# Small inverse transform's four short matmuls: in a row, or one by one between the long matmuls of the first MLP's second layer

## What is computed

```python
X = np.fft.rfft(x, axis=1)                       # x: 4 x 3008 x 256
y = np.fft.irfft(X * (filt_r + 1j * filt_i), n=3008, axis=1)
x = y.reshape(12032, 256)
h = np.maximum(x @ moe_w_in, 0.0)                # 256 x 2048
x = (h * h) @ moe_w_out                          # 2048 x 256
g = x @ moe2_w_gate                              # 256 x 1536
out = (g / (1 + np.exp(-g)) * (x @ moe2_w_val)) @ moe2_w_out
```

## Time and profile before

| what | value |
|---|---|
| median of 3 runs | 2360.11 us (2357.04 to 2362.37) |
| the profiled execution's own time | 2358.64 us |
| its span, first to last instruction | 2356.8 us |
| around the span | 1.84 us |
| mean granted TensorE clock | 0.997 of full speed |
| PE busy | 2329.5 us, 99% of the span |
| PEld busy | 1903.6 us, 81% |
| DVE busy | 1601.1 us, 68% |
| ACT busy | 1272.7 us, 54% |
| s4 jobs | 122, between 94.8 us and 1208.3 us of the span |

### The profile page before, as it was taken

One profiled execution on the slowest core, in us unless ns is written; L12 is line 12 of the kernel. 1 busy time (PEld: TensorE's weight loads), 2 busy tenths in 40 slices (PEclk: granted clock), 3 DMA queues, 4 the chain that ended last, 5 costly groups with the idle time before them and its releaser, 6 DMA issues.

```text
span 2356.8 us, 31292 instructions
## 1 busy us (share of the span) xinstructions
PE 2329.5 (99%) x10581; PEld 1903.6 (81%) x10581; DVE 1601.1 (68%) x2707; ACT 1272.7 (54%) x2468; POOL 61.2 (3%) x124
## 2 busy tenths in 40 slices
PE   8899999999999999999999999999999999999999
PEld 4688888888888888888888878888888888888887
DVE  3567766677666776566555777777777777777776
ACT  4566656566655665555544445555555555555554
POOL 0100000000000000000000000000000000000000
PEclk9899999999999999999999999999999999999999
DMA  9643433333333333101002101001011011010000
GB/s 270 207 132 96 129 96 107 91 107 112 101 98 99 99 106 122 29 27 42 27 19 72 50 1 36 23 14 36 1 36 36 1 36 36 1 36 28 10 19 18
DMA packets 95423, 153.74 MB, mean 65 GB/s; under 512 B 10080, under 2 KB 48416, under 8 KB 94976
## 3 DMA queue, kind: packets, MB, share of 16 engines
q1 hardware_dynamic: 82112, 132.96, 17.9%
q0 software_dynamic: 13152, 18.78, 3.3%
HBM read 101.89 MB, written 49.81 MB: 64 GB/s over the span
## 4 chain that ended last, share of the span: by engine, by line
PE 96%; DMA 2%; SPq 1%; ACT 1%; issue 1%; DVE 1%; POOL 0%; ACTq 0%; DVEq 0%
PE psum L1450 31%; PE psum L1452 31%; PE psum L1451 31%; PE psum L1552 1%; DMA filt0b<-filt 1%; PE psum L1554 1%; PE psum L1461 1%; DMA B_scratch<-b_out 0%; SPq L562 0%; SPq L557 0%; PE psum L1504 0%; DMA w<-w_full 0%; ACT turned L820 0%; DMA A_scratch<-a_out 0%; ACT z_raw L820 0%
## 5 line engine op out<-in xcount | busy, mean ns | idle before, releaser
L1217 DVE SCALAR_TENSOR_TENSOR prod<-psum,act_out 128x512 f32<-128x512 f32 (+1 forms) x384 | 260.9, 679 | 398.4 <-ACT act_out L917 397.9
L917 ACT ACTIVATE act_out<-psum 128x512 f32<-128x512 f32 (+1 forms) x384 | 226.1, 589 | 461.5 <-PE psum L1452 461.2
L1450 PE MATMUL psum<-g_hi,m_hi 128*128 128x512 f32 (+1 forms) x768 | 305.7, 398 | 2.0 <-ACT z_raw L820 1.8
L1450 PE MATMUL psum<-v_hi,m_hi 128*128 128x512 f32 (+1 forms) x768 | 297.7, 388 | 1.5 <-DVE v_lo L1115 1.5
L1452 PE MATMUL psum<-v_hi,m_lo 128*128 128x512 f32 (+1 forms) x768 | 296.7, 386 | 0.0
L1451 PE MATMUL psum<-v_lo,m_hi 128*128 128x512 f32 (+1 forms) x768 | 296.7, 386 | 0.0
L1452 PE MATMUL psum<-g_hi,m_lo 128*128 128x512 f32 (+1 forms) x768 | 296.5, 386 | 0.0
L1451 PE MATMUL psum<-g_lo,m_hi 128*128 128x512 f32 (+1 forms) x768 | 296.4, 386 | 0.0
L1115 DVE TENSOR_TENSOR g_lo<-prod,g_hi 128x512 fp32r<-128x512 f32 (+1 forms) x408 | 270.6, 663 | 1.1 <-ACT g_hi L820 1.0
L820 ACT ACTIVATE g_hi<-prod 128x512 fp32r<-128x512 f32 (+1 forms) x408 | 248.5, 609 | 0.9 <-DVE prod L1251 0.9
L1450 PE MATMUL psum<-g_hi,m_out 128*128 128x512 f32 (+1 forms) x576 | 226.0, 392 | 0.3 <-DVE g_lo L1115 0.3
(11 more groups left out here) (125 smaller groups left out, 4246.9 us busy)
## 6 DMA issues: line engine op xcount, KB each, us to landing
filt_in<-filt SPq DMA_DIRECT2D x36, 512.0 KB, 3.9
z_scratch<-z_raw SPq DMA_DIRECT2D x23, 512.0 KB, 2.9
b_in<-B_scratch SPq DMA_DIRECT2D x122, 96.0 KB, 2.8
zq_raw<-z_scratch SPq DMA_DIRECT2D x44, 256.0 KB, 3.5
B_scratch<-b_out SPq DMA_DIRECT2D x38, 256.0 KB, 2.1
A_scratch<-a_out SPq DMA_DIRECT2D x50, 192.0 KB, 2.1
x_in<-x SPq DMA_DIRECT2D x48, 192.0 KB, 2.8
a_in<-A_scratch SPq DMA_DIRECT2D x36, 256.0 KB, 3.3
```

The costliest lines, as they stand in the source:

```text
L917: nc.scalar.activation(act_out[n % 2][:, 0:w], psum[:, n % 3, 0:w], ACT.Relu).then_inc(relu_done, 1)
L1217: nc.vector.scalar_tensor_tensor(out=prod[n % 2][:, 0:w], in0=psum[:, n % 3, 0:w], scalar=0.0, in1=act_out[n % 2][:, 0:w], op0=ALU.max, op ...
L1450: nc.tensor.matmul(dst, wh, vh, start=start, stop=False, skip_group_check=True)
```

## The change

The four matmuls of an s4 job are no longer issued together between `up1` and `down1`. `down1` gets the job as an argument and issues one of them after each of its own first four matmuls, in the same order as before. The waits that stood ahead of the job stand ahead of its first matmul, that is behind the first matmul of `down1`. The increment of `s4_done` stays on the fourth. Nothing else changes: the same matmuls, operands, banks and semaphores.

```diff
-            def s4(g, c, s3_jobs):
-
-                pe.wait_ge(b_lo_done, g - G0 + 1)
-                pe.wait_ge(w4_loaded[g % 2], 16 * ((g - G0) // 2 + 1))
-                wait(pe, b_copied, s3_jobs)
-                wait(pe, conv_done, s4_count(g, c) - 1)
+            def s4_part(g, c, s3_jobs, k):
+
+                i, low = divmod(k, 2)
+                if k == 0:
+                    pe.wait_ge(b_lo_done, g - G0 + 1)
+                    pe.wait_ge(w4_loaded[g % 2], 16 * ((g - G0) // 2 + 1))
+                    wait(pe, b_copied, s3_jobs)
+                    wait(pe, conv_done, s4_count(g, c) - 1)
                 dst = psum[:, INV, 0:2 * GT].rearrange("p (i h q) -> p i h q", i=PAIR, h=2)
-                for i in range(PAIR):
-                    bh, bl = b_hi[g % 2][:, i, c * P:(c + 1) * P], b_lo[g % 2][:, i, c * P:(c + 1) * P]
-
-                    nc.tensor.matmul(dst[:, i, :, :], bh, w4[g % 2][:, i, :, :], start=True, stop=False,
-                                     skip_group_check=True)
-                    last = nc.tensor.matmul(dst[:, i, 0, :], bl, w4[g % 2][:, i, 0, :], start=False, stop=True,
-                                            skip_group_check=True)
-                last.then_inc(s4_done, 1)
+                if low:
+                    last = nc.tensor.matmul(dst[:, i, 0, :], b_lo[g % 2][:, i, c * P:(c + 1) * P],
+                                            w4[g % 2][:, i, 0, :], start=False, stop=True, skip_group_check=True)
+                else:
+                    last = nc.tensor.matmul(dst[:, i, :, :], b_hi[g % 2][:, i, c * P:(c + 1) * P],
+                                            w4[g % 2][:, i, :, :], start=True, stop=False, skip_group_check=True)
+                if k == 2 * PAIR - 1:
+                    last.then_inc(s4_done, 1)
...
-            def down1(n):
+            def down1(n, s4_job=None, s3_jobs=0):
+
...
-                    last = product(psum[:, ACC + c, 0:w], (w_out1(m1_hi, f, c), w_out1(m1_lo, f, c)),
-                                   (g_hi[n % 4][:, 0:w], g_lo[n % 4][:, 0:w]), f == 0, f == NF1 - 1)
+                    wh, wl = w_out1(m1_hi, f, c), w_out1(m1_lo, f, c)
+                    gh, gl = g_hi[n % 4][:, 0:w], g_lo[n % 4][:, 0:w]
+                    for k, (weights, moving) in enumerate(((wh, gh), (wh, gl), (wl, gh))):
+                        last = nc.tensor.matmul(psum[:, ACC + c, 0:w], weights, moving, start=f == 0 and k == 0,
+                                                stop=f == NF1 - 1 and k == 2, skip_group_check=True)
+                        if s4_job is not None and 3 * c + k < 2 * PAIR:
+                            s4_part(*s4_job, s3_jobs, 3 * c + k)
                 last.then_inc(g_used, 1)
...
-                    s4(*job, s3_jobs)
                     last_s4 = job
                 if n >= HELD:
-                    down1(n - HELD)
+                    down1(n - HELD, job, s3_jobs)
```

## The result

The changed kernel takes 2365.63 us (median of 11 runs, 2364.24 to 2368.86), the kernel before 2360.11 (11 runs, 2356.91 to 2363.86). The ratio is 1.0027, with a 95% interval of 1.0017 to 1.0036: slower by 5.5 us, a little over the 0.2% that a measurement can tell from no change. The forecast was 2363.2 us, in a range of 2352 to 2374.

What follows compares the result with a forecast made beforehand. PE, busy for 99% of the span, was taken to bound the kernel. Loads 0, trail 0 and z stalls +3.1 us on 2358.6 gave 2361.7 us, stated as a median of 2363.2 us, range 2352 to 2374.

Steps and rivals of the forecast that it cites:

- The loads: Four short s4 matmuls among down1's long ones: each still costs a 0.11 us weight load, 0.44 us a job, change 0.
- A: Rival: weight loads of the short matmuls are hidden between down1's long ones, -15.2 us, 2345 us as a median; chance 0.16.
- The stall on z: Where down1 waits for z's copy, the four shorts now come uncovered behind its first matmul: 7 x 0.44 = +3.1 us.
- The trail: Time lost in long matmuls behind the short ones, some 0.03 us a job; taken as unchanged, 0.
- rival B: Alternation in down1: each short unsettles the long one behind it, up to +11 us, 2374 us; chance 0.16.
- The bounds (-3.7 to +11 us): Lost time behind the shorts: gone (-3.7 us), or one such loss for each of four separate shorts (+11 us).
- the point named for B, 1.6 us: Extra loss from alternation in down1 at which the verdict becomes slower: 1.6 us, 0.013 us a job.
- same: Whole kernel: no change beyond the 4.7 us (about 0.2%) a measurement can tell; chance 0.48.
- slower: Whole kernel: slower by over 4.7 us, chances 0.15 and 0.03 from two rivals and 0.14 from the forecast's own case.
- D1 to D6 in 1.58 us: Check in the changed trace: start-to-start from down1's first to sixth long matmul, shorts S1 to S4 between, takes 1.58 us.
- What ends later: The fourth short's s4_done comes 0.9 us later, ACT's part copy 0.27 us; conv keeps 0.2 us margin, cost 0.
- C: Rival: s4_done is seen 0.3 us or more later, so conv, y_lo and s3 move; +3.4 us, 2367 us; chance 0.06.

Runs made afterwards that it cites:

- six_row: Kernel before, shorts still in a row, but each 188-column s4 matmul issued as two of 94 with the same weights: 2383.82 us, ratio 1.0104.
- wide_inter: Changed kernel with each low s4 matmul given all 188 columns instead of 94: 2364.18 us, ratio 1.0021.
- z_row: Changed kernel, but in steps with f = 3 the four short matmuls stand in a row ahead of down1 again: 2362.16 us, ratio 1.0014.
- late_fourth: Changed kernel with the fourth short matmul behind the sixth long matmul of down1 instead of the fourth: 2371.18 us, ratio 1.0049.

## Why the prediction was right, and where it was short

**The loads: right.** "So I cost the four at 0.44 us again": the trace has 0.11 us for each short between long ones, six_row priced two more at 0.21 us a job, and wide_inter showed that columns don't count. A, with its 15 us, is rejected. The Trainium skill, "TensorE: Matmul & The Clock Gate", section "Step-by-step: what each phase is for", says that loads are pulled ahead of matmuls under way when they go to the background buffer. The traces agree, with one such buffer: in none of the 13 does a load start before the matmul right ahead of its own.

**The stall on z: right, 3.1 forecast, 3.3 measured** (7 x 0.47). The 0.03 more in each fits the 0.026 us by which D2 to D4 are longer between shorts. The prediction left out one step, at 252 us of the trace before, whose D4 waits for DVE's copy: there S4 lands behind the wait, 0.1 us. z_row, and the early copy in both kernels, show the cause by taking it away.

**The trail: mis-sized.** "The same number of shorts passes in about the same stretch, so I take 0": it measured 0.02 us a job, 2.3 us. This is rival B's mechanism, a slow long behind each short, at a fifth of its price: B took the whole trail three times more, and only its first interval comes back (0.008 us each), the tail once. It is the 2.3 us that lift the result from the forecast's 2363.2 to 2365.6 and over the 0.2%. The bounds (-3.7 to +11 us) held it, and the point named for B, 1.6 us, was passed. By the sign I was off: "same" had 0.48 and "slower" 0.32, and slower it is, by a small margin. The check that I named, D1 to D6 in 1.58 us, reads 1.61 (522.60 to 524.21), but it could not have shown the trail: with its own trail the old order has 1.61 from S1 to D6 as well, in the mean of 47 jobs, since there all of D1 to D6 stand behind the shorts. In the changed order the tail begins later, and the difference shows from D5 on (523.98 to 525.37, six distances of 0.232 us; before, 0.229 in the mean of 47).

**What ends later: right.** Part starts 1.51 us after `up1` has streamed (forecast 1.49, before 1.21), in the median of the 122 jobs, and conv at 2.04 in both. C cost nothing, and late_fourth shows that 0.45 us more would have cost 5.5 us, through y_lo and x_lo. The prediction priced the margin for y_lo alone.

## What to carry to other kernels

A matmul shorter than a weight load cost its load in every order tried here, and moving it between long matmuls doesn't change that as long as only one load can be ahead; what helps is fewer loads. Before work that PE does during someone else's delay is moved, ask what it covers: four short matmuls ahead of a wait were free in 7 steps, and cost their full price behind it. If a wait is covered by chance, it is better to remove the wait itself, here by one copy placed ahead of two others on ACT.

## What was unexpected of the hardware

A long matmul behind a short one is slower by 4% (0.235 us instead of 0.227), behind a row too, and some ten behind the last short take 0.04 us more together. So singles pay it for each short and a row once; six singles of 94 columns pay more, up to 0.26 us for a long one. Two pairs pay no more than a row (5.920 us against 5.927), and neither the place of the semaphore waits nor the layer plays a part. The operands here are of type float32r (fp32r in the profile); whether other types behave so was not tried.
